# Attention inside a three-stage kernel: the row's own decay left out, the mask added by a matmul, row sums by a column of ones, steps unrolled with four buffers

## What is computed

```python
def _attn_ref(q, k, v, s):
    scale = 1.0 / np.sqrt(D)
    scores = scale * np.matmul(q, k.transpose(0, 1, 3, 2))
    causal = np.triu(np.ones((S, S), dtype=bool), k=1)
    s_pos = np.maximum(s, 0.0)
    cum = np.cumsum(s_pos, axis=-1)
    bias = -(cum[:, :, :, None] - cum[:, :, None, :])
    scores = np.where(causal, -1000000000.0, scores + np.minimum(bias, 0.0))
    scores = scores - np.max(scores, axis=-1, keepdims=True)
    attn = np.exp(scores)
    attn = attn / (np.sum(attn, axis=-1, keepdims=True) + 1e-09)
    return np.matmul(attn, v)
```

## Time and profile before

| what | value |
|---|---|
| median of 3 runs | 1318.68 us |
| profiled execution, span | 1320.4 us |
| TensorE matmul, busy | 1249.8 us (95%) |
| VectorE, busy | 560.1 us (42%) |
| ScalarE, busy | 396.9 us (30%) |
| GpSimd, busy | 109.0 us (8%) |
| mean granted TensorE clock | 0.950 |

### The profile page before, as it was taken

The page is one execution under the profiler, slowest core; times in us unless marked ns, Lnnn a source line. Parts: engine busy times, 40 slices in busy tenths (PEclk is TensorE's granted clock), DMA queues, the critical chain, the costliest instruction groups (busy, mean ns, idle before and its releaser), DMA issues.

```text
span 1320.4 us, 18163 instructions
## 1 busy us (share of the span) xinstructions
PE 1249.8 (95%) x6647; PEld 1110.7 (84%) x6647; DVE 560.1 (42%) x1228; ACT 396.9 (30%) x806; POOL 109.0 (8%) x82
## 2 busy tenths in 40 slices
PE   5799984999999987999999999999999999999999
PEld 4677763788888876899999999999999999999998
DVE  7877866555555454144323323313323323323321
ACT  4565652344444433113212212212212212212211
POOL 2313220111111045000000000000000000000000
PEclk9775885999999997999999999999999999999999
DMA  6243430444444443201101101101101101100000
GB/s 166 63 125 126 154 133 29 172 172 172 172 172 172 172 158 111 89 1 64 65 1 64 64 0 64 64 0 64 64 0 64 64 0 64 64 0 0 24 24 24
DMA packets 20849, 105.45 MB, mean 80 GB/s; under 512 B 4400, under 2 KB 4912, under 8 KB 16720
## 3 DMA queue, kind: packets, MB, share of 16 engines
q1 hardware_dynamic: 14384, 88.51, 19.6%
q0 software_dynamic: 3360, 11.01, 2.9%
q10 hardware_dynamic: 3072, 5.51, 1.2%
HBM read 94.76 MB, written 10.26 MB: 80 GB/s over the span
## 4 chain that ended last, share of the span: by engine, by line
PE 86%; DVE 5%; DMA 4%; issue 2%; ACT 1%; SPq 1%; POOL 0%; DVEq 0%; ACTq 0%; POOLq 0%
PE bank L639 13%; PE bank L638 13%; PE bank L637 13%; PE bank L619 13%; PE bank L621 13%; PE bank L620 13%; PE bank L555 3%; DMA k_raw<-in_kT 2%; PE bank L540 1%; PE bank L528 1%; PE bank L529 1%; PE bank L671 1%; DVE bias L993 1%; DMA x_sb<-x_dram,gather_at 1%; DVE rinv L1016 1%
## 5 line engine op out<-in xcount | busy, mean ns | idle before, releaser
L619 PE MATMUL bank<-xTh,w1h 128*128 128x384 f32 (+1 forms) x1024 | 342.5, 334 | 3.0 <-DVE xTl L1079 1.6
L621 PE MATMUL bank<-xTh,w1l 128*128 128x384 f32 (+1 forms) x1024 | 340.2, 332 | 0.0
L620 PE MATMUL bank<-xTl,w1h 128*128 128x384 f32 (+1 forms) x1024 | 340.2, 332 | 0.0
L848 ACT ACTIVATE hh<-bank 128x384 fp32r<-128x384 f32 (+1 forms) x256 | 123.4, 482 | 653.2 <-PE bank L621 650.5
L639 PE MATMUL bank<-w2h,hl 128*128 128x512 f32 (+1 forms) x768 | 303.2, 395 | 0.0
L638 PE MATMUL bank<-w2l,hh 128*128 128x512 f32 (+1 forms) x768 | 302.0, 393 | 0.0
L637 PE MATMUL bank<-w2h,hh 128*128 128x512 f32 (+1 forms) x768 | 300.9, 392 | 0.0
L1100 DVE SCALAR_TENSOR_TENSOR hl<-bank,hh 128x384 fp32r<-128x384 f32 (+1 forms) x256 | 139.5, 545 | 367.3 <-ACT hh L848 363.3
L619 PEld LDWEIGHTS bank<-xTh,w1h 128*128 128x128 f32 x1024 | 193.3, 189 | 5.5 <-issue 2.0
L620 PEld LDWEIGHTS bank<-xTl,w1h 128*128 128x128 f32 x1024 | 193.4, 189 | 1.2
L621 PEld LDWEIGHTS bank<-xTh,w1l 128*128 128x128 f32 x1024 | 193.3, 189 | 0.0
(11 more groups left out here) (172 smaller groups left out, 791.3 us busy)
## 6 DMA issues: line engine op xcount, KB each, us to landing
raw<-in_w SPq DMA_DIRECT2D x16, 2048.0 KB, 8.6
raw<-in_w1b SPq DMA_DIRECT2D x8, 2048.0 KB, 7.6
raw<-in_w2b SPq DMA_DIRECT2D x8, 2048.0 KB, 7.9
q_raw<-in_qT SPq DMA_DIRECT2D x16, 288.0 KB, 6.1
k_raw<-in_kT SPq DMA_DIRECT2D x16, 288.0 KB, 7.5
cumj<-cum_dram SPq DMA_DIRECT2D x8, 576.0 KB, 5.7
y_dram<-x_sb ACTq DMA_DIRECT2D x16, 256.0 KB
x_dram<-x_sb SPq DMA_DIRECT2D x1, 2304.0 KB, 9.4
```

Of the source, the lines that this page charges most:

```text
L619: pe.matmul(dst, w1h[:, c, fs], xTh[:, c, ts], start=(c == 0), stop=False)
L620: pe.matmul(dst, w1h[:, c, fs], xTl[:, c, ts], start=False, stop=False)
L621: mm = pe.matmul(dst, w1l[:, c, fs], xTh[:, c, ts], start=False, stop=(c == DC - 1))
L848: act.activation(hh[:, f, 0:n_cols], bank[:, f % UP_BANKS, 0:n_cols], ACT.Relu).then_inc(st.hh_ready, 1)
```

## The change

- The row's own `cum` is not subtracted any more: `decay`, `cumi`, `cumi_now`, `take_rows`, the buffer `bias` and the six first transposes of `cum` go. `logits` adds the column's `cum` (`cumj`) to the scores directly.
- The mask is added in PSUM: `scores` gets a third matmul, identity times mask, for the 128 columns of the diagonal block (64 for t = 4).
- v gets a column of ones on either side (`VW` = 130), so `mix` makes 65 columns, of which one is the row's sum. `exponentials` reads no accumulator, and `finish` takes the sums from PSUM, in two instructions.
- `copy_turned` of the tiles t = 3 and t = 4 is VectorE's; t = 0 to 2 stay ScalarE's.
- The loops over pairs of heads are unrolled to 80 written steps. TensorE: `scores(k + 5)`, `turn(k + 2)`, `mix(k)`. ScalarE: `exponentials(k + 3)`, `copy_turned(k + 1)`. VectorE: `copy_turned(k + 1)`, `logits(k + 5)`, `finish(k - 1)`. `neg`, `prob`, `probT` and `negmax` have four slots, v and cum three heads. The scores keep two PSUM slots and so do the transposes.
- The high parts are made in steps 6 and 7 of a head instead of 8 and 9.
- SP issues, for head h, q and k when the low parts of head h - 2 are made, cum when the logits of head h - 3 are done, v when `mix` of head h - 3 is done. `gates`, `raw1` and `raw2` are loaded behind the loads of head 4.

```diff
+        HIGH_STEPS = (6, 7)
+        SCORES_AHEAD, EXP_AHEAD, TURN_AHEAD, COPY_AHEAD = 5, 3, 2, 1
+        def by_dve(k):
+            return ORDER[k % HEAD][1] >= ST - 1
...
-                    sp.wait_ge(head_done, 4 * it + (2 * w + 2 + 4))
-                    load_v(h + 2, w)
-                    load_cum(h + 2, w)
-                    if not last or w == 0:
-
-                        sp.wait_ge(qk_low, 4 * it + (2 * w + 4))
-                        load_qk(h + 3, 1 - w)
+            for h in range(2, H):
+
+                sp.wait_ge(qk_low, 2 * (h - 2) + 2)
+                load_qk(h)
+                if h >= CUM_RING:
+                    sp.wait_ge(logits_ready, HEAD * (h - CUM_RING + 1) + 2)
+                load_cum(h)
+                if h >= V_RING:
+                    sp.wait_ge(mixed, HEAD * (h - V_RING + 1) + RING)
+                load_v(h)
+                if h == 4:
+                    for c, g in enumerate((wg, wn, gate2)):
+                        sp.dma_start(gates[:, :, c * E:(c + 1) * E], g).then_inc(gates_loaded, 16)
+                    sp.dma_start(raw1[:], w1[0]).then_inc(SP_.raw1_loaded, 16)
+                    sp.dma_start(raw2[:], w2[0]).then_inc(SP_.raw2_loaded, 16)
...
                     pe.matmul(dst[:, c0:c1], q, k_h[w][:, u * S + c0:u * S + c1], start=True, stop=False)
+                    if c1 == width:
+                        pe.matmul(dst[:, t * P:width], ident_r[:, outs], mask_r[:, rows.stop - nrow:rows.stop], start=False, stop=False)
                     mm = pe.matmul(dst[:, c0:c1], q, k_l[w][:, u * S + c0:u * S + c1], start=False, stop=True)
...
-                    mm = pe.matmul(bank[rows, OUT_BANK[u, w], t * HD:(t + 1) * HD],
-                                   probT[0:wide, k % 2, j * nrow:(j + 1) * nrow],
-                                   v_sb[0:wide, w, j, HD * u:HD * u + HD], start=(j == 0), stop=(j == t))
+                    mm = pe.matmul(bank[rows, OUT_BANK[u, h % 2], t * (HD + 1):(t + 1) * (HD + 1)],
+                                   probT[0:wide, k % RING, j * nrow:(j + 1) * nrow],
+                                   v_sb[0:wide, w, j, (HD + 1) * u:(HD + 1) * (u + 1)], start=(j == 0), stop=(j == t))
...
+            for k in range(ALL):
+                if k + SCORES_AHEAD < ALL:
+                    scores(k + SCORES_AHEAD)
+                if k + TURN_AHEAD < ALL:
+                    turn(k + TURN_AHEAD)
+                mix(k)
...
-                               bias=negmax[rows, k % 2:k % 2 + 1], scale=-1.0,
-                               accum_out=sums[rows, head % 4, t:t + 1]).then_inc(prob_ready, 1)
+                               bias=negmax[rows, k % RING:k % RING + 1], scale=-1.0).then_inc(prob_ready, 1)
...
-                v.tensor_tensor_reduce(out=neg[rows, k % 2, 0:width], in0=src[:, 0:width], in1=bias[rows, k % 2, 0:width],
+                v.tensor_tensor_reduce(out=neg[rows, k % RING, 0:width], in0=src[:, 0:width], in1=cumj[rows, w, u, 0:width],
...
-                v.tensor_scalar(inv, sums[:, head, :], EPS, None, ALU.add).then_inc(sums_own, 1)
+                src = bank[:, OUT_BANK[u, h % 2], 0:STEPS * (HD + 1)].rearrange("p (t d) -> p t d", d=HD + 1)
+                total, value = (src[:, :, 0], src[:, :, 1:1 + HD]) if u == 0 else (src[:, :, HD], src[:, :, 0:HD])
+                v.tensor_scalar(inv[:, 0:ST], total[:, 0:ST], EPS, None, ALU.add).then_inc(sums_own, 1)
+                v.tensor_scalar(inv[rows, ST:ST + 1], total[rows, ST:ST + 1], EPS, None, ALU.add).then_inc(sums_own, 1)
...
+            for k in range(ALL):
+                if k + COPY_AHEAD < ALL and by_dve(k + COPY_AHEAD):
+                    copy_turned(k + COPY_AHEAD)
+                if k + SCORES_AHEAD < ALL:
+                    logits(k + SCORES_AHEAD)
+                if k and (k - 1) % HEAD in LAST:
+                    finish(k - 1)
+            finish(ALL - 1)
```

More of the change, by code:

```diff
@@ L558, in mix @@
                 mm.then_inc(mixed, 1)
-            pe.wait_ge(cumT_done, 2)
-            def attend(it, last):
-                for k in range(BODY):
-                    if not last or k + 3 < BODY:
-                        scores(it, k + 3)
-                    if not last or k + 1 < BODY:
-                        turn(it, k + 1)
-                    mix(it, k)
-            for k in range(3):
-                scores(0, k)
-            turn(0, 0)
-            with pe.Fori(0, LOOPS - 1) as it:
-                attend(it, False)
@@ L574, in _ @@
-            attend(LOOPS - 1, True)
+            pe.wait_ge(const_ready, 6)
+            pe.wait_ge(mask_ready, 2)
+            for k in range(SCORES_AHEAD):
+                scores(k)
+            for k in range(TURN_AHEAD):
+                turn(k)
+            for k in range(ALL):
[4 more added lines that the diff above has]
+                mix(k)
             def turn_token(st, t, src):
@@ new lines, in copy_turned, with high_part @@
+            def copy_turned(k):
+                u, t, rows, nrow, width = step(k)
+                act.wait_ge(probT_done, k + 1 + RING)
+                act.wait_ge(mixed, k + 1)
+                whole = (t + 1) * nrow
+                act.copy(probT[:, k % RING, 0:whole], bank[:, TURN_BANK + k % 2, 0:whole]).then_inc(probT_by_act, 1)
+            def high_part(h, i):
+                to, raw = ((q_hl[h % 2], q_raw), (k_h[h % 2], k_raw))[i]
+                act.wait_ge(qk_loaded[h % 2], 64 * (h // 2) + 64)
+                act.copy(to, raw[:, h % 2]).then_inc(qk_high, 1)
@@ new lines, in _ @@
+            high_part(0, 0)
+            high_part(0, 1)
+            for k in range(EXP_AHEAD):
+                exponentials(k)
+                if k < COPY_AHEAD and not by_dve(k):
+                    copy_turned(k)
+            for k in range(ALL):
+                if k + EXP_AHEAD < ALL:
+                    exponentials(k + EXP_AHEAD)
+                if k + COPY_AHEAD < ALL and not by_dve(k + COPY_AHEAD):
+                    copy_turned(k + COPY_AHEAD)
+                h = k // HEAD
+                if k % HEAD in HIGH_STEPS:
+                    i = HIGH_STEPS.index(k % HEAD)
+                    if h + 2 < H:
+                        high_part(h + 2, i)
+                    else:
+                        act.wait_ge(SP_.raw1_loaded, 16)
+                        c = 2 * (h + 2 - H) + i
+                        act.copy(w1h[:, c, :], raw1[:, c, :]).then_inc(SP_.w1h_ready, 1)
@@ L997, in logits @@
[L997 to L1002 removed]
+            v.wait_ge(const_ready, 6)
+            v.tensor_copy(ident_r[:], ident[:]).then_inc(mask_ready, 1)
+            v.tensor_copy(mask_r[:], maskneg[:]).then_inc(mask_ready, 1)
+            link(v.tensor_copy(rinv[:].rearrange("p a b -> p (a b)"), ones[:, 0:2 * STEPS]))
@@ new lines, in copy_turned @@
+            def copy_turned(k):
+                u, t, rows, nrow, width = step(k)
+                v.wait_ge(probT_done, k + 1 + RING)
+                v.wait_ge(mixed, k + 1)
+                whole = (t + 1 if t < ST else ST) * nrow
+                last = v.tensor_copy(probT[:, k % RING, 0:whole], bank[:, TURN_BANK + k % 2, 0:whole])
+                if t == ST:
+                    last = v.tensor_copy(probT[0:HALF, k % RING, whole:whole + nrow], bank[0:HALF, TURN_BANK + k % 2, whole:whole + nrow])
+                last.then_inc(probT_by_dve, 1)
@@ L1024, in finish @@
                                 inv[:, 0:ST].unsqueeze(2).to_broadcast([P, ST, HD]), ALU.mult)
[L1025 removed]
+                v.tensor_tensor(x_sb[rows, ST:ST + 1, at:at + HD], value[rows, ST:ST + 1, :],
                                 inv[rows, ST:ST + 1].unsqueeze(2).to_broadcast([HALF, 1, HD]),
                                 ALU.mult).then_inc(head_done, 1)
[L1029 to L1040 removed]
```

320 lines of the change are left out of this document (116 added, 204 removed).

## The result

The kernel after takes 1273.65 us (median, 1271.95 to 1277.35), the one before 1319.13 in the same rounds: a ratio of 0.9669 over the rounds, 95% interval 0.9640 to 0.9698, in which the quotient of the two medians, 0.9655, lies too. The forecast was 1278 in a range of 1263 to 1306, the case the likeliest of the five. The profiled execution of after has a span of 1271.7 us, and its attention ends at 139.0 us (end of the last `L957`, the last `x_sb`) in place of 184.9. Of the 48.7 us between the two spans 45.9 lie in attention and 2.8 behind it.

The account below looks back on a forecast made before the run. Attention bounded by TensorE's idle time and low clock: 20.5 start + 111.3 heads + 5.5 clock rise + 5 small waits + 1.5 last `finish` = 143.8 us instead of 184.9, so 1278, range 1263 to 1306.

Parts of the forecast that it names:

- What bounds it, and the level of the clock: Attention: idle time at each head's end, then 10 to 25 us at half clock; afterwards TensorE is the longest engine.
- 16.2 us of waits for q and k: ScalarE's high part in attention: five waits for q and k, 16.2 us in total, go with earlier issue by SP.
- three things that make the idle time: TensorE at a head's end: late q and k, VectorE instructions held by GpSimd, VectorE's load of 16.2 of 21 us.
- only just hidden: Loads at h = 4: 4.2 MB ahead of head 5's q and k, about 20 us against 21; uncovered, 1 to 5 us once.
- bounds of 0.41 and 0.7: VectorE's turned copies of t = 3 and 4: 0.6 us taken per step, 32 steps, 19 us, 2.4 per head.
- that rival: New wait per head, from a reciprocal held by GpSimd or late q and k: 21 us instead of 5, 1294; chance 0.12.
- 15.0 + 13 = 28: ScalarE in attention: accumulator reads (15.0 us) and 32 large copies (13 us) go, leaving 8.9 us per head.
- 14.3: A head's TensorE time at the high clock: 13.2 us of present work plus 1.1 for mask matmuls.
- The clock's rise: Start of attention: 12 us at the low level before the clock rises, costing 5.5 us.
- Small waits: Attention: 5 us over all heads for waits that the longer leads do not cover.
- the 140 to 150: Sign of a right forecast: attention's last `x_sb` comes at 140 to 150 us.
- the rival by which the clock never rises: TensorE's clock stays low through attention: heads of 26.4 us, +47.5 us, 1366 in all; chance 0.05.

Follow-up runs that it names:

- b1_qk_early: Kernel before, with SP issuing q and k of head h+3 before waiting for `head_done`; ratio to before 0.9972, gain 3.7 us.
- a4_mask_thrice: Kernel after, with the mask matmul made three times in each step instead of once; ratio to before 0.9816, gain 24.3 us against after's 43.6.
- a6_one_late_load: Kernel after, with q and k of head 6 alone issued late, after the second step of head 4; ratio to before 0.9706.
- a2_short_lead: Kernel after, with the shorter leads of before and the high parts back in steps 8 and 9, four buffers kept; ratio to before 0.9759.
- a5_copies_by_act: Kernel after, with all turned copies on ScalarE again; ratio to before 0.9681.
- a7_warm_start: Kernel after, with 52 transposes of the identity on TensorE ahead of the first scores; ratio to before 0.9683.
- a9_mask_by_dve: Kernel after, with VectorE adding the mask to the cum tile for each head's second unit, 40 of 80 mask matmuls gone; ratio to before 0.9783.
- b3_early_no_decay: Kernel before, with early q and k and without decay, mask left out, leads and two buffers kept; ratio to before 0.9699.
- a1_qk_late: Kernel after, with q and k of head h (from 3 on) issued only after `head_done` of head h-3; ratio to before 0.9777.

## Why the prediction was right, and where its terms were off

**What bounds it, and the level of the clock: right.** Three pieces come close to the trace. The first is the clock, which costs only where TensorE is busy. The stretches of before at 0.50, from 20.5 us on, added up:

```profile
sum 85.90, PE 75.97 PEld 62.68 DVE 65.92 ACT 43.99 POOL 29.22; mean PE 9.50 PEld 7.84 DVE 8.24 ACT 5.50 POOL 3.65
```

So TensorE was busy for 76.0 of the 85.9 us, and in after for 5.0 of its 5.9. At half speed (0.22 us between starts for 0.11) the 71.0 us between them lose 35.5; by the rates of 24.2 and 13.2 us per head, 0.45 each, 32. The second is the waits: TensorE was idle for 21.4 us of 164.2 before and is for 1.8 from 20.5 to 139.0, 19.6 less. The third is the mask, which takes 9 back. Together 43 to 46, measured 45.9. The clock is the larger part.

**The parts: right together, not one by one.** The prediction put 16.2 us of waits for q and k down as a part that goes. That was misread: 6.9 of them are the wait for the first q and k, which stays, and 9.3 were there to go. Gone alone, in b1_qk_early, they are worth 3.7. The prediction called them, the held instructions and VectorE's load three things that make the idle time, and didn't say that each would keep the clock low by itself. As the whole change was forecast, and from TensorE's rates at the two levels, neither did harm to the number; a forecast of one part would have failed.

**The loads: right.** The 4.2 MB that go ahead of q and k of head 5 were called only just hidden, with 1 to 5 us once if not. In after the high part's one wait from 20 us on, 1.5 us, ends at 77.1 us in the fourth head, where the high part of head 5 is made, and TensorE is idle for none of it (4.00 of 4.00 us busy from 76 to 80).

**VectorE.** The copies took 17.6 + 3.3 = 20.9 us where 19 was taken: 0.65 for each step, inside the bounds of 0.41 and 0.7 and nearer to the upper. (The 7.5 us off `finish` are 7.2 by the prediction's own terms, 0.9 per head either way.) The reciprocal took 0.19 us all 16 times, eight of them while GpSimd's instruction ran, so the lower bound held and that rival falls. From 0 us to the end of attention VectorE's busy time went from 139.5 to 83.7 us, 55.8 less, where 8 x 7.4 = 59 had been worked out.

**ScalarE.** The same view gives 104.0 and 80.9: 23.0 less, where 15.0 + 13 = 28 were subtracted. The step that failed is subtracting a group's busy us from an engine's. Groups count each instruction from its own start to its own end, and neighbours overlap: before, ScalarE's groups sum to 120.9 us in 104.0 busy us, and an accumulator read begins before its exponential ends. It did not matter, as ScalarE had room: from 20.5 to 137.4 us, 7.95 heads, it is busy 9.5 us per head where 8.9 had been put, and VectorE 9.2 where 8.8.

**TensorE.** The mask matmul's 0.11 us is what a4_mask_thrice shows (0.105). A head takes 14.7 us and not 14.3; 0.4 x 7.8 is 3 us too little. The 13.2 of it were taken from a single stretch of 10 us, less than a head; that it lacked the slower steps is an argument.

**The clock's rise: over-sized.** 12 us at the low level were taken from a fall in the earlier trace rows, 5.0 were there (20.5 to 25.5), so the term is 2.3 us and not 5.5. It isn't fixed either: in the profiled runs that begin as after does the rise came between 25.2 (a6_one_late_load) and 35.5 us (a2_short_lead). In a5_copies_by_act it came at 34.3, and 8.8 us more at the low level, 4.0 lost, are most of the 5.0 by which its attention ends later than after's. In before the low stretches within attention lasted 6.8 to 30.7 us, a wider spread than the 10 to 25 that the prediction read.

**Small waits: over-sized.** 5 us were put in, and TensorE was idle for 0.25 us up to 137.4 and 1.5 at the last step. Behind attention 1132.7 us in place of 1135.5, inside the 3 us allowed; the runs give 1132.7 to 1137.6 there with the same code, so this is spread.

In sum: head +3, rise -3.2, small waits and last step -4.8, together -5, and 143.8 became 139.0. So the nearness of the number owes something to errors that offset each other, and the end of attention lies 1 us outside the 140 to 150 that the prediction had named as a sign. With the -2.8 behind attention the span is 7.6 below the forecast's; the median lies 2.0 above the span, where 1.7 below it had been put, and so only 4.3 below.

**The rule on transposes.** Beside the rival by which the clock never rises the prediction names the Trainium skill ("TensorE: Matmul & The Clock Gate", "Part 4: PE-mode transpose"), which says that transposes do not count in the same way as work that lifts the clock. a7_warm_start contradicts it for these: the granted clock went to 1.00 behind 5.8 us of nothing but fp32 transposes. The measurement decides. That these run in the mode the page speaks of is taken from the code's `transpose`; the trace records them as matmuls. The Trainium skill's rule on the shared SBUF interface ("VectorE: DVE Perf Modes", "Two Vector instructions with no wait between them") agrees with a9_mask_by_dve, where the instruction with two SBUF tensors is stretched from 0.29 to 2.08 us and the neighbouring `L942`, with one and the PSUM, keeps its 0.42.

## What to carry to other kernels

When TensorE's clock falls at a recurring gap, count the causes that can each make that gap before pricing any of them: here they gave 4 and 13 us alone and 40 together, and one 3.6 us wait costs 5 us. Read waits from the stretch that the change can touch: a wait at the start of the kernel sits in the same total. Idle time in pieces of under a microsecond mostly cost only itself, so leads that cut one long wait into short ones pay twice: here they brought 12 us, while moving copies off ScalarE, which already waited, brought nothing. And idle time on VectorE is not free for instructions with two SBUF inputs wherever GpSimd is at work.

## What the runs showed of the hardware

- Idle time in pieces and idle time at one place are not the same to the clock. a2_short_lead had TensorE idle for 9.7 of 117.7 us, never over 0.83 at once, b3_early_no_decay for 8.7 of 122.1, up to 0.7 at once while the clock was up, and neither fell; a6_one_late_load was idle for 2.2 us about one wait and fell for 6.8 us. Yet a1_qk_late fell at 54.2 us for 3.4 us behind a single idle 0.86 us, and did not behind one of the same length at 122.4, and a9_mask_by_dve did not fall behind 1.0 us at one place in each of six heads. What decides isn't settled.
- fp32 transposes of 128x128 alone lifted the clock at 7.7 us, from 0.21 us each to 0.11.
- A GpSimd instruction of 2.65 us held VectorE's `tensor_tensor` with two SBUF inputs (2.08 us in place of 0.29), and the 16 that ran beside one of GpSimd's took 0.96 us or more, the 24 others 0.29 or less. In after, none of the eight reciprocals that met one was held (0.19 us, from SBUF to SBUF), nor were the logits or copies that read PSUM (0.42 us for 128x256 with GpSimd at work or not).
